# Attention and two feed-forward layers on one core: second buffers for the first nine items, another PSUM bank for one turn, and new places in the order of steps

## The reference

```python
q, k, v: (4, 8, 576, 64) float32                 # batch, heads, positions, head width
scores = q @ k^T / 8, masked unless position//64 of the row >= that of the column
attn   = exp(scores - rowmax) / (rowsum + 1e-9)
x      = (attn @ v), heads side by side: (2304, 512)
h = x @ w_in                                     # (512, 2048)
g = h if h >= 1; 0 if h <= -1; (h + 1)**2 / 4 between
x2 = g @ w_out                                   # (2048, 512)
h2 = x2 @ w2_in;  g2 = h2 * cos(h2);  out = g2 @ w2_out
```

## Time and profile before

| | us |
|---|---|
| median of 3 runs (1099.52 to 1102.16) | 1101.63 |
| the profiled execution | 1110.2 |
| its span, first to last instruction | 1108.2 |
| PE busy | 1015.8 (92% of the span) |
| DVE, ACT, POOL busy | 657.7, 596.2, 411.2 |
| mean granted TensorE clock | 0.993 |

### The profile page before, as it was taken

One profiled execution on the slowest core, in us unless ns is written; L12 is line 12 of the kernel. 1 busy time (PEld: TensorE's weight loads), 2 busy tenths in 40 slices (PEclk: granted clock), 3 DMA queues, 4 the chain that ended last, 5 costly groups with the idle time before them and its releaser, 6 DMA issues.

```text
span 1108.2 us, 19878 instructions
## 1 busy us (share of the span) xinstructions
PE 1015.8 (92%) x7360; PEld 946.0 (85%) x7360; DVE 657.7 (59%) x1420; ACT 596.2 (54%) x1230; POOL 411.2 (37%) x446
## 2 busy tenths in 40 slices
PE   4578789999898999898999999999999999999997
PEld 3377689888898889898889999899999999999996
DVE  4557566666665666566664238765655656556563
ACT  5557566666665566655653236654554544444443
POOL 3447555545445444544542222122222222222221
PEclk9999899999999999999999999999999999999999
DMA  3314321121121111111111014301101001011000
GB/s 129 113 55 160 102 74 61 55 80 54 63 70 48 64 68 48 65 69 46 65 53 39 20 55 162 127 1 38 38 0 38 13 25 38 0 38 38 0 20 20
DMA packets 30886, 62.28 MB, mean 56 GB/s; under 512 B 3680, under 2 KB 11872, under 8 KB 30816
## 3 DMA queue, kind: packets, MB, share of 16 engines
q1 hardware_dynamic: 29664, 57.16, 16.1%
q10 hardware_dynamic: 1152, 4.19, 0.9%
HBM read 51.90 MB, written 9.44 MB: 55 GB/s over the span
## 4 chain that ended last, share of the span: by engine, by line
PE 72%; DVE 11%; ACT 6%; issue 5%; POOL 3%; DMA 2%; ACTq 0%; POOLq 0%; DVEq 0%; SPq 0%
PE hidden L1012 31%; PE acc L1029 17%; PE acc L1037 10%; PE turned L958 5%; PE heads_out L975 4%; PE scores L944 3%; PE scores L945 2%; DVE pt_lo L769 2%; DVE work L830 2%; DVE neg_max L752 1%; POOL wout_lo L491 1%; ACT probs L570 1%; ACT pt_hi L579 1%; POOL probs L466 1%; DVE win_lo L808 1%
## 5 line engine op out<-in xcount | busy, mean ns | idle before, releaser
L497 POOL TENSOR_TENSOR g_lo<-work,g_hi 128x512 fp32r<-128x512 f32 x144 | 188.5, 1309 | 413.7 <-ACT g_hi L662 413.5
L1012 PE MATMUL hidden<-x_hi,win_hi 128*128 128x256 f32 x1152 | 329.0, 286 | 4.0 <-DVE x_lo L824 1.9
L1012 PE MATMUL hidden<-x_lo,win_hi 128*128 128x256 f32 x1152 | 323.3, 281 | 0.0
L1012 PE MATMUL hidden<-x_hi,win_lo 128*128 128x256 f32 x1152 | 323.2, 281 | 0.0
L1012 PEld LDWEIGHTS hidden<-x_hi,win_hi 128*128 128x128 f32 x1152 | 217.9, 189 | 8.9 <-issue 3.4
L1012 PEld LDWEIGHTS hidden<-x_lo,win_hi 128*128 128x128 f32 x1152 | 217.9, 189 | 3.4
L1012 PEld LDWEIGHTS hidden<-x_hi,win_lo 128*128 128x128 f32 x1152 | 220.1, 191 | 0.0
L466 POOL TENSOR_SCALAR probs<-probs,row_inv 64x576 f32<-64x576 f32 (+2 forms) x160 | 95.3, 599 | 252.9 <-DVE row_inv L764 252.8
L1037 PE MATMUL acc<-g_hi,wout_hi 128*128 128x256 f32 x576 | 168.2, 292 | 11.1 <-POOL wout_lo L491 11.1
L1037 PE MATMUL acc<-g_lo,wout_hi 128*128 128x256 f32 x576 | 161.6, 281 | 0.0
L1037 PE MATMUL acc<-g_hi,wout_lo 128*128 128x256 f32 x576 | 161.4, 280 | 0.0
(11 more groups left out here) (63 smaller groups left out, 1834.5 us busy)
## 6 DMA issues: line engine op xcount, KB each, us to landing
qk_raw<-qk_late SPq DMA_DIRECT2D x32, 448.0 KB, 3.3
qk_raw<-qk_early SPq DMA_DIRECT2D x32, 256.0 KB, 2.6
v_raw<-v_late SPq DMA_DIRECT2D x32, 160.0 KB, 3.3
x_raw<-x_scratch SPq DMA_DIRECT2D x9, 512.0 KB, 3.5
out<-y_stage SPq DMA_DIRECT2D x36, 128.0 KB, 2.4
x_raw<-w_in SPq DMA_DIRECT2D x8, 512.0 KB, 3.5
y_stage<-w_out SPq DMA_DIRECT2D x8, 512.0 KB, 3.6
x_scratch<-y_stage ACTq DMA_DIRECT2D x8, 512.0 KB, 2.7
```

Source lines behind the costliest of these rows:

```text
L497: nc.gpsimd.tensor_tensor(g_lo[:, m % G_RING, :], work[:, m % 2, :], g_hi[:, m % G_RING, :], ALU.subtract).then_inc(g_lo_made, 1)
L1012: last = nc.tensor.matmul(into, w[:, p, c, half * P:(half + 1) * P], x[:, c, :], start=(i == 0), stop=(i == len(products) - 1))
```

## The change

It has four parts.

1. Items 1, 3, 5 and 7 (`apart`) get buffers of their own, lent by feed-forward buffers that are not yet in use: q, k and the turned probabilities in `g_hi` and `g_lo`, scores in the two banks of `acc`, turned and weighed values in the two banks of `hidden`, `part_sum` in `work`, v in the unused part of `v_parts`. Every wait that guards a reuse now names the item before last for items 0 to 8 (`user_before`).
2. A late item's second turn goes into the bank `heads_out` instead of `turned`. It waits for the `add` of the item before; its third turn waits for `pt_lo` of the first.
3. The places of splits and loads of the first layer's weights are two tables, `SPLIT_AT` and `LOAD_AFTER` (a place up to 9 is after that many items, 10+u is the end of unit u of tile 0). At the start v and the second item's q and k are loaded ahead of the first weights.
4. Nearly all of `AT` has other numbers, and an item alone has 9 slots instead of 10.

```diff
-SLOTS = (10, 11, 19)
+SLOTS = (9, 11, 19)
-    "score": (0, 0, 0), "score_c": (0, 0, 7), "turn": (7, 10, 11), "turn_b": (0, 0, 15),
-    "turn_c": (0, 0, 19), "weigh": (14, 16, 21), "k_hi": (-8, -7, -8), "q_hi": (-5, -8, -6),
-    "v_hi": (6, 5, 7), "exp": (1, 3, -1), "exp_b": (2, 3, 4), "exp_c": (0, 0, 9),
-    "pt_hi": (8, 10, 10), "pt_hi_b": (0, 0, 13), "pt_hi_c": (0, 0, 15), "move": (12, 16, 23),
-    "q_lo": (-4, -7, -4), "max": (0, 1, -2), "max_b": (0, 1, 3), "max_c": (0, 0, 7),
-    "inv": (0, 3, 3), "inv_b": (1, 4, 6), "inv_c": (0, 0, 11), "pt_lo": (8, 13, 12),
-    "pt_lo_b": (0, 0, 15), "pt_lo_c": (0, 0, 17), "add": (12, 19, 23), "k_lo": (-6, -8, -8),
-    "norm": (0, 2, -3), "norm_b": (2, 2, 4), "norm_c": (0, 0, 9), "v_lo": (7, 6, 8),
+    "score": (0, 0, 0), "score_c": (0, 0, 7), "turn": (8, 13, 11), "turn_b": (0, 0, 16),
+    "turn_c": (0, 0, 19), "weigh": (14, 19, 22), "k_hi": (-7, -9, -8), "q_hi": (-1, -8, -8),
+    "v_hi": (1, 6, 6), "exp": (1, 0, 2), "exp_b": (1, 3, 3), "exp_c": (0, 0, 7),
+    "pt_hi": (10, 11, 13), "pt_hi_b": (0, 0, 14), "pt_hi_c": (0, 0, 15), "move": (14, 15, 22),
+    "q_lo": (-1, -7, -4), "max": (1, 0, 0), "max_b": (1, 0, 2), "max_c": (0, 0, 7),
+    "inv": (2, 2, 3), "inv_b": (2, 4, 6), "inv_c": (0, 0, 11), "pt_lo": (11, 12, 15),
+    "pt_lo_b": (0, 0, 17), "pt_lo_c": (0, 0, 19), "add": (17, 19, 23), "k_lo": (-2, -9, -11),
+    "norm": (0, 3, -2), "norm_b": (0, 3, 2), "norm_c": (0, 0, 7), "v_lo": (9, 6, 6),
+def apart(n):
+    return n < ALONE and n % 2 == 1
+def user_before(n):
+    return n - 2 if n < ALONE else n - 1
-def weights_beside(t, u):
-    if t or u % 4 not in (1, 3):
-        return None
-    which, pair = (0, u // 4 + 3) if u % 4 == 1 else (1, u // 4 + 1)
-    return (which, pair) if pair < PAIRS else None
-WEIGHTS_ALONE = {1: (0, 0), 3: (0, 1), 5: (1, 0), 6: (0, 2)}
-FIRST_AFTER = {2: [(0, 1)], 4: [(0, 2)], 7: [(1, 1)], 8: [(0, 3)], 10: [(0, 4)], 11: [(1, 2)], 12: [(0, 5), (1, 3)],
-               13: [(0, 6)], 14: [(1, 4), (0, 7)], 15: [(1, 5)], 16: [(1, 6)], 18: [(1, 7)]}
+SPLIT_AT = ((1, 3, 8, 10, 13, 18, 20, 26), (6, 11, 16, 18, 24, 27, 30, 34))
+LOAD_AFTER = ((-1, 0, 3, 9, 9, 11, 12, 13), (-1, 9, 10, 12, 13, 15, 16, 17))
+def weights_at(place):
+    return [(which, pair) for which in range(2) for pair in range(PAIRS) if SPLIT_AT[which][pair] == place]
+def loads_after(n):
+    return [(which, pair) for pair in range(1, PAIRS) for which in range(2) if LOAD_AFTER[which][pair] == n]
...
+        def pt_hi_of(n):
+            return g_hi[:, 2, :] if apart(n) else pt_hi
+        def turned_of(n, e):
+            return hidden[:, 0, :] if apart(n) else heads_out if e == 1 else turned
+        def bank_of(n, i):
+            if apart(n):
+                return acc[:, i:i + 1, 0:ext_of(i)]
...
             load_qk(0)
+            load_qk(1)
+            load_v(0)
+            load_v(1)
             load_first(0, 0)
-            load_v(0)
-            load_qk(1)
-            load_v(1)
             load_first(1, 0)
...
             def split_k_hi(n):
-                if n:
-                    act.wait_ge(scores_made, first_tile(n))
+                if user_before(n) >= 0:
+                    act.wait_ge(scores_made, first_tile(user_before(n) + 1))
...
             def turn(n, e):
-                if turn_n:
-                    pe.wait_ge(pt_lo_made, turn_n)
+                if e == 1:
+                    pe.wait_ge(heads_read, n)
+                elif e == 2:
+                    pe.wait_ge(pt_lo_made, first_turn(n) + 1)
+                elif user_before(n) >= 0:
+                    pe.wait_ge(pt_lo_made, first_turn(user_before(n) + 1))
```

More of the change, by code:

```diff
@@ L407, in _ @@
                 after_split(n)
-                for which, pair in FIRST_AFTER.get(n, ()):
+                for which, pair in loads_after(n):
                     load_first(which, pair)
@@ L511, in tile @@
                             attention(n, k)
-                        w = weights_beside(t, u)
-                        if w and w[0] == 1:
-                            split_wout(w[1])
+                        for which, pair in weights_at(ALONE + 1 + u) if t == 0 else ():
+                            if which == 1:
+                                split_wout(pair)
                     s = made_in.get(u)
@@ L527, in _ @@
                     attention(n, k)
-                w = WEIGHTS_ALONE.get(n)
-                if w and w[0] == 1:
-                    split_wout(w[1])
+                for which, pair in weights_at(n + 1):
+                    if which == 1:
+                        split_wout(pair)
             hidden_lo(0, 0)
@@ L574, in turned_hi @@
                 act.wait_ge(turned_made, first_turn(n) + e + 1)
-                if e == 0 and n:
-                    act.wait_ge(heads_made, n)
+                if e == 0 and user_before(n) >= 0:
+                    act.wait_ge(heads_made, user_before(n) + 1)
                 source, place = turned_tiles(n, e)
-                nc.scalar.activation(place(pt_hi), source, ACT.Copy).then_inc(pt_hi_made, 1)
+                nc.scalar.activation(place(pt_hi_of(n)), source, ACT.Copy).then_inc(pt_hi_made, 1)
             def move_part(n):
@@ L719, in _ @@
                     attention(n, k)
-                w = WEIGHTS_ALONE.get(n)
-                if w:
-                    split_w(*w)
+                for which, pair in weights_at(n + 1):
+                    split_w(which, pair)
             split_x(0, False)
@@ L768, in turned_lo @@
                 source, place = turned_tiles(n, e)
-                nc.vector.tensor_tensor(place(pt_lo), source, place(pt_hi), ALU.subtract).then_inc(pt_lo_made, 1)
+                nc.vector.tensor_tensor(place(pt_lo_of(n)), source, place(pt_hi_of(n)), ALU.subtract).then_inc(pt_lo_made, 1)
             def add_parts(n):
@@ L776, in add_parts @@
                         dve.wait_ge(x_lo_made, 2 * (tile - X_RING + 1))
-                    last = nc.vector.tensor_tensor(place, heads_out[half_rows(n), first:first + cols],
-                                                   part_sum[half_rows(n), first:first + cols], ALU.add)
+                    last = nc.vector.tensor_tensor(place, heads_out_of(n)[half_rows(n), first:first + cols],
+                                                   part_sum_of(n)[half_rows(n), first:first + cols], ALU.add)
                 last.then_inc(heads_read, 1)
@@ L910, in _ @@
                     attention(n, k)
-                w = WEIGHTS_ALONE.get(n)
-                if w and w[0] == 0:
-                    split_win(w[1])
+                for which, pair in weights_at(n + 1):
+                    if which == 0:
+                        split_win(pair)
             split_x(0, False)
@@ L943, in score @@
                 for into, first, end in pieces:
-                    nc.tensor.matmul(into, q_tile, k_hi[:, first:end], start=True, stop=False)
-                    last = nc.tensor.matmul(into, q_tile, k_lo[:, first:end], start=False, stop=True)
+                    nc.tensor.matmul(into, q_tile, k_hi_of(n)[:, first:end], start=True, stop=False)
+                    last = nc.tensor.matmul(into, q_tile, k_lo_of(n)[:, first:end], start=False, stop=True)
                 last.then_inc(scores_made, 1)
@@ L973, in weigh @@
                 for j, at, first in parts:
-                    for buf in (pt_hi, pt_lo):
-                        last = nc.tensor.matmul(heads_out[:, first:width], v_parts[:, j, :, :].rearrange("p a d -> p (a d)"),
-                                                buf[:, at + first:at + width], start=(j == 0 and buf is pt_hi),
-                                                stop=(j == parts[-1][0] and buf is pt_lo))
+                    for low, buf in enumerate((pt_hi_of(n), pt_lo_of(n))):
+                        last = nc.tensor.matmul(heads_out_of(n)[:, first:width],
+                                                v_of(n)[:, j, :, :].rearrange("p a d -> p (a d)"),
+                                                buf[:, at + first:at + width], start=(j == 0 and low == 0),
+                                                stop=(j == parts[-1][0] and low == 1))
                 last.then_inc(heads_made, 1)
```

85 lines of the change are left out of this document (48 added, 37 removed).

## The result

The changed kernel takes 1062.43 us (median of 4 runs, 1061.84 to 1064.54) against 1100.58 for the kernel before (4 runs): a ratio of 0.966 with a 95% interval of 0.9635 to 0.9678. It is inside the predicted range (1062.0 to 1092.0), but only by 0.4 us: 26.3 us were forecast and 38.2 came. That it still falls inside is luck; all three terms of the sum were too small. Its profiled execution took 1062.99 us.

A forecast was written before the change was run, and what follows sets the result against it. PE, busy 1015.8 of 1108.2 us, was taken as the bound, with waits to win in three stages. Gains of 3.0 (items alone), 11.9 (tile 0 to 205 us) and 11.4 (late items) made 1101.6 - 26.3 = 1075.3 us, range 1062 to 1092.

The forecast's parts named there:

- The items alone: Before the first feed-forward matmul: plain period 5.15 us instead of 5.21, cheaper w_in splits; 3.0 us gained, bounds 0 and 6.8.
- The chain: Items alone: second maximum at T+1.84, then hops over `pt_lo`, `move`, `q_hi` and `q_lo` to the next score, 5.15 us.
- Tile 0 and after: Tile 0 and the stretch to 205 us: 13.9 - 5.0 + 3.0 = 11.9 us gained, bounds 5 and 25.5.
- the long dip of the clock: Tile 0, after the 4.68 us w_out wait: lower clock for some 5.6 us, costing 2.8, expected to go.
- The term for the loads: Tile 0: with one staging buffer, late loads make ACT stand 8.4 us in all; 5.0 charged.
- The `weigh` waits: Tile 0: 2.0 of 7.9 us of `weigh` and `turn` waits gained; behind it, 1.0 of 3.7.
- Late items: From 205 to 600 us: 17.8 us of turn waits go, 6.4 come instead; 11.4 us gained.
- The 6.4 us that were to come instead: Late items: later `pt_lo_c` before `weigh` and shorter run-up of `exp_b` and `exp_c`, 0.2 us for each of 32 items.
- The rule of the port: Items alone: a DVE instruction with two SBUF inputs contends with GpSimd reading SBUF; 0.17 us per item, sum stays 3.0.
- Slower, `move` ahead of its `weigh`: Rival, items 9 to 31: ACT stands about 2 us at `move`, holding up what follows; 1121 us at full size, chance 0.07.
- The waits move: Rival, all three stages: removed waits come back at the next place; only 10 us gained, 1091.6 us, chance 0.24.
- nearly all goes: Rival, all three stages: nearly every wait goes and ACT's standing is harmless; about 40 us gained, 1062 us, chance 0.11.

The follow-up runs named there:

- e10_before_places: The kernel before with the new places of weight splits and loads alone, one w_out split a unit later: 1096.4 us, ratio 0.995 to the kernel before.
- e3_old_places: The changed kernel with the first layer's weight splits and loads back at the old places: 1080.6 us, ratio 0.979 to the kernel before.
- e8: The changed kernel with one added wait: for a late item POOL starts `k_lo` only when `q_lo` is done; 1111.6 us, ratio 1.0095 to the kernel before.
- e2b_single_v9: The changed kernel with items 0 to 8 on single buffers and their `v_hi` moved from slot 1 to 9: 1064.0 us, ratio 0.965 to the kernel before.

## Why the prediction was right, and where it was short

**The stages and what bounds each.** Right: all the gain lies in the three named stages, and no experiment gives the second layer any of it. PE's idle time from its first feed-forward matmul to the end of tile 6 was to fall from some 53 to some 30 us; it fell from 52.6 to 24.7.

**The items alone: 3.0 forecast, 4.6 came.** The chain was right hop by hop. In the changed kernel, from a score at 25.63: second maximum done at +1.87 (forecast 1.84), `pt_lo` to `move` 1.77 (1.77), `move` to `q_hi` 0.40 (0.40), the period 5.09 (5.15). Off were the periods with splits. "Second buffers alone do not make it overlap more" is shown:

| first feed-forward matmul at | old order | new order |
|---|---|---|
| single buffers | 57.6 (57.8 with the new places, e10_before_places) | 59.3 (52.55 with `v_hi` moved) |
| second buffers | 58.3 | 53.05 |

The prediction missed that the new order makes `v_hi` wait on a single buffer; it did not look at what the new places would cost without the buffers.

**Tile 0 and after: 11.9 forecast, 17.0 came.** The waits for w_out and the long dip of the clock went, as said (the dip was worth 3.4 us and not 2.8). The term for the loads was mis-sized: ACT stood 4.5 us for w_out, 2 times, where 8.4 in five places were counted, and 5.0 of that were charged to PE. The count took ACT to be at a split when PE ends the unit; it probably comes later, which no run here shows by itself. The `weigh` waits were mis-sized the other way round: 3.0 of 11.6 were counted as gained, while the wait for `pt_lo` or `norm` is 6.5 in tile 0 and 0 in tile 1. That is the order's work, as e3_old_places shows, whose tile 1 lasts 63.7 with the old places. And the sum took places and order as two terms that add up:

| tile 0 | old order | new order |
|---|---|---|
| old places | 93.7 | 98.4 |
| new places | 91.3 | 82.6 |

Each alone is worth -4.7 or 2.4, both 11.1 (the new order is here with its buffers and its bank). The table has the clock in it. PE's idle time is 19.1 and 20.7 us in the upper row and 16.1 and 10.3 in the lower; the lower level of the clock costs 3.4 and 8.5, 5.1 and 0. So the order alone hardly changes the idle time, and its -4.7 is the clock's.

**Late items: 11.4 forecast, 17.8 came.** That the four-piece turns stop waiting is right. That the five-piece ones do is wrong: their 2.3 us were counted as gained, and seven of them wait 3.7. The 6.4 us that were to come instead were put in the wrong place: `weigh` waits 0.2 us for `pt_lo` and scores for `exp` fell from 5.5 to 2.6. What came is `q_lo`, from 2.3 to 7.5 us, with a dip of the clock behind each of its two longest waits, and the prediction listed it as something that would get better. The rule of the port that it cites was applied to the items alone and found harmless there; it bites in the late items, where POOL's instructions are twice as long and follow each other. Here too the parts do not add up:

| tiles 2 to 6 | old order | new order |
|---|---|---|
| turn in `turned` | 392.7 | 430.3 |
| second turn in `heads_out` | 379.3 | 374.9 |

The bank is worth 13.4 us in the old order and 55.4 in the new; the new order by itself costs 37.6. Why the late items won more than the 11.8 us by which their waits fell is settled only in part: PE's idle time in tiles 2 to 6 fell by 16.4, from 29.0 to 12.6, which includes gaps that no wait is named for, and the last 1.4 us stay open. The clock has no part in it, as it cost 3.4 us before and after.

**The rivals.** "Slower, `move` ahead of its `weigh`" did not happen: ACT waits 0.3 us for `heads_out` in tile 0 (1.9 before). "The waits move" is right for `q_lo` and wrong in size. The outcome, 1062.4, is the figure of "nearly all goes" (1062), which was given 0.11; the forecast was 1075.3.

## What to carry to other kernels

In a hand-ordered program like this one a buffer, a bank and an order are not terms to be added: of three pairs tried here each had a half that was worth little or cost up to 37.6 us without the other, so an edit is priced against the order that it comes with. A freed buffer should be asked which instruction stands earlier because of it; where the answer is one instruction, moving that one may do as well. Where a subtraction of two SBUF operands on VectorE is on the critical chain, look at what GpSimd runs beside it, and give GpSimd a pause there: one added wait was worth 7 us here. When two traces of such kernels are compared, the stretches at the lower clock should be counted apart from the idle time, or a stage is credited with what the clock did.

## What the runs showed of the hardware that was not expected

- A DVE instruction with both inputs in SBUF, met by POOL instructions that follow each other without a gap, does not get in between them: 0.49 us became up to 3.22, and in the three pictures above it ended 0.34 to 0.35 us after the last of them. POOL's own instructions, which came first there, were hardly lengthened (`k_lo` 1.40 to 1.42 us, against 1.40 in e8, where nothing ran against it).
- The granted clock fell or stayed with the same waits: behind a wait of 2.21 us for `exp` it was at the lower level for some 3.4 us in the trace of the kernel before, and not at all in that of e10_before_places. A wait of 1.83 us in the changed kernel was followed by such a stretch, a wait of 2.20 us in the kernel before was not. In tile 0, `weigh` waits 2.19 us in the changed kernel and 2.18 in e2b_single_v9, and only the second is followed by one.
- Tile 8 and the second layer, the same code in all kernels, lasted either about 444 or about 451 us. In 100 us of it, with PE busy throughout and the granted clock at 1.00, PE ran 645 matmuls in the trace of the kernel before and 654 in that of the changed one. What decides between them stays open.

```profile
800.00:900.00 100.00, 100.00 (x645) 90.81 (x644) 58.22 (x78) 47.66 (x76) 23.41 (x18) 1.00 0.07 21
```

```profile
760.00:860.00 100.00, 100.00 (x654) 90.96 (x653) 59.08 (x81) 48.63 (x77) 24.04 (x19) 1.00 0.08 21
```
